# Expert stage pipelined by one tile, with the relu rows turned through DRAM and VectorE instead of on TensorE

## What is computed

```python
kv = einsum('bhsd,bhse->bhde', k, v);  out = einsum('bhsd,bhde->bhse', q, kv)     # 8 batches, 8 heads, 576 x 64
x = out / sqrt(mean(out * out) + 1e-6) * g_norm                                  # -> 4608 tokens x 512
x = square(maximum(x @ w_in, 0)) @ w_out                                         # 512 -> 2048 -> 512
logits = x @ w_gate + modality_bias[modality_id];  e_idx = argmax(logits)        # 8 experts
for e in range(8):                                                               # top-1 routing
    mask = e_idx == e
    out[mask] = gate_w[mask, None] * (maximum(x[mask] @ w1[e], 0) @ w2[e])       # 512 -> 1024 -> 512
```

## Time and profile before

| | |
|---|---|
| runs | 1524.31, 1524.43, 1529.36 us; median 1524.43 |
| profiled execution | span 1524.2 us, 24645 instructions; it has no time of its own beside the span |
| TensorE busy | 97% of the span |
| VectorE, ScalarE, GpSimd busy | 41%, 33%, 24% |
| DMA | 236.42 MB, mean 155 GB/s |
| expert stage | from 1011.6 us to the end |

### The profile page before, as it was taken

The page is one execution under the profiler, slowest core; times in us unless marked ns, Lnnn a source line. Parts: engine busy times, 40 slices in busy tenths (PEclk is TensorE's granted clock), DMA queues, the critical chain, the costliest instruction groups (busy, mean ns, idle before and its releaser), DMA issues.

```text
span 1524.2 us, 24645 instructions
## 1 busy us (share of the span) xinstructions
PE 1478.5 (97%) x7915; PEld 1301.5 (85%) x7916; DVE 619.1 (41%) x1538; ACT 498.7 (33%) x927; POOL 365.0 (24%) x377
## 2 busy tenths in 40 slices
PE   6899999999999999999999999988999999999998
PEld 5788998988999998999898999876888888888886
DVE  3363635445554535453636464422222222222222
ACT  2343433433433333433333433321222222222222
POOL 2452312121312122222222131202222222222221
PEclk8999999999999999999999999999999999999999
DMA  6633655563656463464655354754875112751170
GB/s 155 162 101 118 171 173 162 154 183 92 201 123 209 106 194 123 153 170 156 162 171 160 111 180 151 217 199 156 319 284 182 41 41 78 268 213 41 47 255 21
DMA packets 192772, 236.42 MB, mean 155 GB/s; under 512 B 92287, under 2 KB 107039, under 8 KB 192674
## 3 DMA queue, kind: packets, MB, share of 16 engines
q1 hardware_dynamic: 185122, 215.18, 46.1%
q0 software_dynamic: 7552, 20.03, 3.9%
HBM read 148.14 MB, written 88.07 MB: 155 GB/s over the span
## 4 chain that ended last, share of the span: by engine, by line
PE 85%; DMA 6%; DVE 3%; issue 3%; POOL 2%; ACT 1%; SPq 1%; DVEq 0%; POOLq 0%; ACTq 0%
PE ps_y L810 15%; PE ps_h L810 14%; PE ps_h L632 7%; PE ps_y L632 7%; PE ps_h L634 7%; PE ps_h L633 7%; PE ps_y L634 7%; PE ps_y L633 7%; PE ps_a L668 2%; PE ps_b L695 2%; PE ps_b L717 2%; DMA stage<-in_moe_w_in 2%; DMA w_lo<-stage 1%; PE ps_c L755 1%; PE ps_y L823 1%
## 5 line engine op out<-in xcount | busy, mean ns | idle before, releaser
L543 POOL TENSOR_TENSOR stage<-stage,stage_hi 128x512 f32<-128x512 f32 x128 | 167.6, 1309 | 652.9 <-ACT stage_hi L922 575.0
L1203 DVE TENSOR_TENSOR g_sb<-relu_sb 128x384 f32<-128x384 f32 x192 | 131.5, 685 | 400.1 <-ACT relu_sb L979 395.5
L632 PE MATMUL ps_h<-xT_hi,weights 128*128 128x384 f32 x768 | 268.6, 350 | 5.8 <-POOL weights L535 3.2
L634 PE MATMUL ps_h<-xT_hi,weights 128*128 128x384 f32 x768 | 260.3, 339 | 0.0
L633 PE MATMUL ps_h<-xT_lo,weights 128*128 128x384 f32 x768 | 259.9, 338 | 0.0
L632 PE MATMUL ps_y<-weights,g_hi 128*128 128x512 f32 x576 | 233.8, 406 | 0.3 <-DVE g_lo L1208 0.3
L634 PE MATMUL ps_y<-weights,g_lo 128*128 128x512 f32 x576 | 227.2, 394 | 0.0
L633 PE MATMUL ps_y<-weights,g_hi 128*128 128x512 f32 x576 | 226.0, 392 | 0.0
L979 ACT ACTIVATE relu_sb<-ps_h 128x384 f32<-128x384 f32 x192 | 93.8, 488 | 317.3 <-PE ps_h L634 304.9
L810 PE MATMUL ps_y<-weights,xT_hi 128*128 128x512 f32 x640 | 183.7, 399 | 0.0
L810 PE MATMUL ps_h<-weights,xT_hi 128*128 128x512 f32 x640 | 172.2, 391 | 1.4 <-DVE xT_lo L1106 1.4
(11 more groups left out here) (169 smaller groups left out, 1735.8 us busy)
## 6 DMA issues: line engine op xcount, KB each, us to landing
stage<-in_moe_w SPq DMA_DIRECT2D x128, 256.0 KB, 2.9
w_hi<-stage_hi SPq DMA_DIRECT2D x128, 256.0 KB, 2.8
w_lo<-stage SPq DMA_DIRECT2D x128, 256.0 KB, 3.2
weights<-w_hi SPq DMA_DIRECT2D x32, 1024.0 KB, 6.5
weights<-w_lo SPq DMA_DIRECT2D x32, 1024.0 KB, 6.6
rows<-y_sb SPq DMA_DIRECT2D x13, 774.0 KB, 4.9
k_sb<-in_k SPq DMA_DIRECT2D x60, 144.0 KB, 3.2
v_sb<-in_v SPq DMA_DIRECT2D x30, 288.0 KB, 4.0
```

The lines of the kernel that those rows point to most:

```text
L543: pool.tensor_tensor(stage[n % 2][:, :], stage[n % 2][:, :], stage_hi[n % 2][:, :].bitcast(F32), ALU.subtract).then_inc(piece_lo, 1)
L632: pe.matmul(out_ap, lhs[0], rhs[0], start=start, stop=False)
L634: return pe.matmul(out_ap, lhs[1], rhs[0], start=False, stop=stop)
L1203: dve.tensor_tensor(g_sb[:, :], relu_sb[:, :], relu_sb[:, :], ALU.mult).then_inc(g_done, 1)
```

## The change

What it does, part by part:

1. **Turning h.** `transpose_h` and its four-by-two transposes a tile are gone from TensorE. ScalarE's relu now writes its 512 columns in another order, and ScalarE issues a store of that half to a DRAM buffer `h_dram[half]` (256 KB, runs of 512 bytes) and then a load back (256 KB, 2 KB a partition), which together exchange blocks of rows and columns. VectorE then transposes the 32 x 32 blocks of the 128 x 512 half in one instruction (`turn_h`), and `h_hi` and `h_lo` read that from SBUF instead of PSUM, through a permuted view.
2. **Pipelining.** TensorE's order is hidden(T + 1), output(T) where it was hidden(T), output(T). There is one buffer for the turned h, so `h_hi(T)` waits for output(T - 1). `transpose_rows(T + 1)` now stands in hidden(T), six matmuls before its end. On VectorE `x_lo(T + 1)` stands behind the turn of the first half of tile T, and `scale(T - 1)` behind the turn of the second half. The metadata pass through one more buffer (`meta_mid`).
3. **GpSimd** scatters tile T - 3 where it scattered T - 2, ahead of passing the rows of tile T.
4. **Early tiles and the least number.** `EARLY` goes from 2 to 3, and each expert has at least `LEAST` = 2 tiles. For these inputs: 3 + (2, 2, 3, 13, 3, 10, 2, 3) = 41 tiles, since expert 0 keeps 430 - 384 = 46 tokens for its own tiles and gets 2.
5. **Unrolling.** The loop over pairs of experts becomes eight copies of the code. The waits for weights are one expert's w1 ahead of its first hidden and its w2 behind the first output of that round; expert 1's w2 is loaded without a wait once the lists are in.

The core of the diff (the names and counts of semaphores that follow from it are left out):

```diff
-EARLY = 2
+EARLY = 3
+LEAST = 2
...
+            for e in range(E):
+                n_tiles, previous = tiles_of(eng, e), tile_before(eng, e)
+                at_tile(previous, e, 0)
+                with eng.Fori(1, n_tiles) as t:
+                    at_tile(previous + t, e, t)
...
+            def load_w1(e):
+                if e > 1:
+                    sp.wait_ge(h_ps, tile_before(sp, e - 1) * 2 + (GROUPS * CH + 2))
...
+            def load_w2(e):
+                if e > 1:
+                    sp.wait_ge(y_ps, tile_before(sp, e - 1) + (GROUPS + 1))
...
-            def transpose_h(T, half):
-                pe.wait_ge(relu_done, T * 2 + half + 1)
-                for k_ in range(4):
-                    last = pe.transpose(chunks(ps_hT[half][:, :])[:, k_, :],
-                                        relu_B[half][:, k_ * P:(k_ + 1) * P], ident[:, :])
-                last.then_inc(hT_ps, 1)
...
+            def hidden_of(T, n, at=lambda place: None, rows=True):
                 pe.wait_ge(x_lo_done, T + (ROWS + 1))
                 hidden(n, 0, 0, 6)
                 hidden(n, 0, 6, 3 * KC)
+                hidden(n, 1, 0, 6)
+                if rows:
+                    transpose_rows(T + 1)
+                hidden(n, 1, 6, 3 * KC)
+            def output_of(T, n, at=lambda place: None):
                 pe.wait_ge(y_by_dve, T + GROUPS)
                 pe.wait_ge(hT_lo_done, T * 2 + 1)
+                output(n, 0, 12)
                 pe.wait_ge(hT_lo_done, T * 2 + 2)
+                output(n, 12, 3 * FC)
...
+            hidden_of(0, 0, first_places)
+            hidden_of(1, 0, second_places)
+            output_of(0, 0, second_places)
+            hidden_of(2, 0, third_places, rows=False)
+            output_of(1, 0)
+            transpose_rows(3)
...
+                with pe.Fori(1, n_tiles) as t:
+                    hidden_of(previous + t + 1, e % 2)
+                    output_of(previous + t, e % 2)
+            output_of(last_tile(pe), (E - 1) % 2)
...
+            def store_h(T, half):
+                act.wait_ge(relu_done, T * 2 + half + 1)
...
+                act.dma_start(h_dram[half].rearrange("a p r -> p a r"),
+                              relu_B[half].rearrange("p (a r) -> p a r", a=4)).then_inc(h_out[half], 16)
+            def load_h(previous, half):
+                act.wait_ge(h_out[half], previous * 16 + 32 if previous is not None else 16)
...
+                act.dma_start(h_swapped[half], h_dram[half].rearrange("a (t b) r -> (a t) (b r)", b=4)).then_inc(h_in[half], 16)
...
+                dve.transpose(h_turned[half], h_swapped[half]).then_inc(hT_done, 1)
...
-                act.wait_ge(hT_ps, T * 2 + (half + 1))
+                act.wait_ge(hT_done, T * 2 + (half + 1))
+                act.wait_ge(y_ps, T + GROUPS)
+                act.activation(h_chunks(0, half), turned_chunks(half), ACT.Copy).then_inc(hT_hi_done, 1)
```

More of the change, by code:

```diff
@@ L99, in routed_mlp_program @@
     rows_dram = nc.dram_tensor("rows", [N + 1, ROW], F32, kind="Internal").ap()
+    h_dram = [nc.dram_tensor(f"h_rows{half}", [4, P, P], F32, kind="Internal").ap() for half in range(2)]
     lists_dram = nc.dram_tensor("lists", [EARLY * P + E * LIST, 1], F32, kind="Internal").ap()
@@ L180, in routed_mlp_program @@
         relu_B = [kv_sb[n][:, :, :].rearrange("p a b -> p (a b)") for n in range(2)]
+        h_swapped = [stage_hi[half][:, :].bitcast(F32) for half in range(2)]
+        h_turned = [xn[:, :], tile_T[:, :, :].rearrange("p k t -> p (k t)")]
         W = KC * F
@@ L1001, in relu @@
                 act.wait_ge(h_ps, T * 2 + (GROUPS * CH + half + 1))
-                act.activation(relu_B[half], ps_h[half][:, :], ACT.Relu).then_inc(relu_done, 1)
-            def h_hi(T, half):
-                act.wait_ge(hT_ps, T * 2 + (half + 1))
-                act.activation(h_B[0][:, 4 * half:4 * half + 4, :], chunks(ps_hT[half][:, :]),
-                               ACT.Copy).then_inc(hT_hi_done, 1)
-            def tile(T, e2, n, t):
-                for half in range(2):
-                    relu(T, half)
-                    h_hi(T, half)
-                x_hi(T + 1)
+                if not isinstance(T, int) or T:
+                    act.wait_ge(h_out[half], T * 16)
@@ L1016, in _, with tile @@
+            def tile(previous, e, t, rows=True):
+                T = previous + 1
+                relu(T, 0)
+                store_h(T, 0)
+                relu(T, 1)
+                store_h(T, 1)
+                load_h(previous, 0)
+                if rows:
+                    x_hi(T + 1)
+                load_h(previous, 1)
+                h_hi(T, 0)
+                h_hi(T, 1)
             last_group = Group(0, GROUPS - 1)
             other("yT", 0, None, last_group, True)
+            other("yT", 1, None, last_group, True)
@@ L1018, in _ @@
             relu(0, 0)
-            other("yT", 1, None, last_group, True)
-            h_hi(0, 0)
+            store_h(0, 0)
             other("yT", 2, None, last_group, True)
             relu(0, 1)
+            store_h(0, 1)
+            x_hi(1)
+            load_h(None, 0)
+            load_h(None, 1)
+            other("argmax", 0, None, last_group, True)
+            h_hi(0, 0)
             h_hi(0, 1)
-            other("argmax", 0, None, last_group, True)
-            x_hi(1)
-            for T in range(1, EARLY):
-                tile(T, None, None, None)
+            tile(0, None, None)
@@ L1028, in _ @@
+            tile(1, None, None, rows=False)
+            x_hi(3)
             act.wait_ge(tiles_done, 1)
-            all_experts(act, None, tile)
+            all_experts(act, tile)
         @block.vector
```

274 lines of the change are left out of this document (131 added, 143 removed).

## The result

The changed kernel takes **1685.43 us** (median of 4 runs, 1677.77 to 1695.34), the kernel before beside it 1525.0 us (4 runs): a ratio of **1.105**, 95% interval 1.1004 to 1.1088. The forecast was 1598 us, with a range of 1535 to 1650: slower, as said, but by 160 us and not by 74. The profiled execution took 1677.77 us, its span is 1676.0.

The account below looks back on a forecast made before the run. TensorE's instructions set the pace before; with the change, loops through DRAM would. 1060 to hidden(3) + 190 (11.7 tiles beside weights) + 25.3 x 12.33 = 312 + 10 (clock) + 26 (end) = 1598 us, range 1535 to 1650.

Parts of the forecast that it names:

- 11.36 us of TensorE work: Expert stage: TensorE's own work a tile falls from 12.31 us to 11.36 once two of three transpose groups go.
- Period without weights, 12.33: Loop tiles without weight traffic: 12.33 us each, bounds 11.7 to 13.2, so these tiles gain nothing.
- loop A: Path over x_lo: hidden, relu, half 0's store and load, turn, x_lo, next hidden; 9.42 us plus the load's time.
- loop B: Path over the rows: half 1's store, load, turn, scale, scatter, row copy, row transposes; 6.93 us plus store and load.
- Trips beside weights, +2.0 each: Stores and loads of h while weights stream: 2.0 us longer each, bounds 0 and 3.6, making a tile 16.3 us.
- the 11.7 tiles: Loop tiles run while weights load: 190 us in all at 16.3 us a tile.
- rival 3: Deeper stalls: trips beside weights as slow as the pieces, 19.9 us a tile, 10.8 tiles, 1659 us in all; chance 0.16.
- Clock, 10 us: TensorE's clock halves behind long waits beside weights, adding at most 1.8 us a tile; half taken, 10 us in all.
- Early tiles, h(3) at 1060: Before the loop: hidden(3), whose start is h(3), begins at 1060, losing about 4 us.
- The end, 26.3: From the start of hidden(40), h(40), to the end: 26.3 us, as the last output waits for its own round trip.
- Rival 1: ScalarE's trips aren't slowed by the weights: all 37 periods at 12.33 us, 1540 us in all; chance 0.20.
- Rival 2: Round trip hidden, TensorE's 11.36 us the period: 1502 us; needs store plus load (S + L) at most 4.43; chance 0.07.

Follow-up runs that it names:

- e1: The changed kernel with expert 2 to 7's weight pieces cut from 1 MB to 64 KB, so nearly no weight traffic: 1605.81 us.
- e5: The changed kernel with x_hi ahead of the loads on ScalarE, and x_lo, the metas and scale ahead of both turns on VectorE: 1610.3 us.
- e6: e5 with the weight pieces of experts 2 to 7 cut to 64 KB: 1524.2 us.
- e12: e5 with the edits of e7 and e8, and the weight pieces of experts 2 to 7 cut to 64 KB: 1516.42 us.
- e2: The changed kernel with x_hi ahead of the loads on ScalarE, and x_lo and the metas ahead of the turns on VectorE: 1673.43 us.
- after: The changed kernel itself, without further edits: 1685.43 us, 1.105 times the kernel before.
- e13: e5 with each 1 MB weight piece of experts 2 to 7 as two DMAs of 512 KB, still two in flight: 1588.94 us.
- e8: e5 with expert 1's w2 fetched ahead of the token lists and tile 3's x_hi and x_lo ahead of tile 2's h: 1605.9 us.
- e7: e5 with VectorE's turned halves written to two free PSUM banks instead of SBUF: 1596.1 us.

## Why the prediction was right in direction and wrong in size

The miss is 1676.0 - 1598 = 78 us of span: 4.9 ahead of h(3), 69.7 in the 37 periods (581.7 against 190 + 312 + 10), 3.2 behind h(40). The 69.7 can be split in two ways. By e1, 50 are in the loop without weights and 20 in what the weights add. By kind, TensorE's waits are 115.8 us where the forecast's terms leave 82 (512 - 420.3 - 10), and its work is 45.5 us slower where 10 were set down: 34 and 35.5. So the loops were too short in the sum, and the clock term was too small; each is half of the miss.

- **What bounds the kernel; 11.36 us of TensorE work.** Right: 11.4 in e5, e6 and e12.
- **The chain is the question, not the sum of work.** Right. VectorE is at 42%; its 0.71 us turn was taken as 0.69.
- **Period without weights, 12.33.** This step failed first, and is the larger part. The structure was right (A and B, of nearly equal length; e2), but the sum let B, 12.33, be the longer, and A is what TensorE waits for. In the tile shown loop A takes 12.99 us where the sum gave 9.42 + 2.6 = 12.02: +7.78 to the load's issue for 7.25 (TensorE's hidden takes 6.24 behind a wait, not 5.92; the steps in the queue are longer than 0.08), 2.98 from the load's issue to VectorE's release for 2.6 (half 1's loads alone do land after 2.6; half 0's goes out 0.7 us behind half 1's store), and 0.1 until VectorE starts. Then the mean: in e1, without weight traffic, it is 13.7: half 0's load takes 3.3 us to its turn in the median and up to 5.7, as trips also meet GpSimd's row transfers and each other, and two loops without slack let each such delay through. What delays a single trip is read from the order of transfers, not isolated by a run; e6 shows that with slack nearly none of it reaches TensorE (0.3 us of waits in its 37 periods). 37 x (13.67 - 12.33) = **50 us**, of which 30 are waits and 20 slower work of TensorE. The bound of 13.2 was there, and was still too low for a mean.
- **Trips beside weights, +2.0 each.** Failed: the stores behind a group of pieces take 5.1 to 7.9 us in after's chain, and half 0's loads up to 9.2 (8.74 and 7.20 in e5's), up to 5 or 6 more than in quiet. The bound "as slow as a piece, 6.5" was exceeded. That a trip waits for the pieces ahead of it and then makes its own fits the tile shown and e13, but no run shows it alone. With it the 11.7 tiles failed: 19 periods are long, 17 with pieces in flight, since each expert comes as two groups of pieces, and a group touches more than one tile. But the long tile itself, 17.9 us with its slower work, is between the forecast's 16.3 (without it) and rival 3's 19.9. In all the weights cost 76 us (after less e1) where 190 + 10 - 11.7 x 12.33 = 56 were forecast: **20 us**. Of these 20, 16 are slower work and only 4 are waits (50 against 46): the longer trips don't add up so far, since their waits fall on one tile and spare the next (6.2, 3.4, 9.0 and 1.6 us in the four from h(4) on), and the mean wait of a long tile is 4.7 us where 16.3 - 11.36 = 4.9 were forecast. That this comes out so near is luck.
- **Clock, 10 us.** Right in kind: 0.50 behind a long wait. Failed in size: it costs 35 us in the 37 periods. The step that failed is "In loop B only 1.83 us of TensorE's work lies on the path, so a halved clock adds at most 1.8 us a tile". That holds for loop B; in loop A, which TensorE waits for, the whole of hidden is on the path, and hidden(5) takes 9.12 us of work for 6.06, 3.1 more. And it comes in 15 stretches, where 11.7 tiles were reckoned. Some 10 us more of slower work stand at full clock, about 0.3 behind each wait; nothing here says why.
- **Early tiles, h(3) at 1060.** 1064.9, and near by luck: the last logits, from which the forecast counts, come 8.5 us earlier in this run than before (1012.13 for 1020.65), in code that the change doesn't touch. From there to h(3) are 52.7 us and not 39.4: 31.7 for 28.2 to the turned ids, 21.0 for 11.2 behind them. Named there: the row transposes, the round trip, the ids. Not named: ScalarE's loads for tile 2 stand ahead of tile 3's `x_hi`, and half 1's load is issued only when its store has landed beside expert 1's w2. e8, which sets both right, takes 12.5 us behind the ids, but its ids come later by nearly as much.

```profile
1012.13 0.96 PE L717 MATMUL ps_b<-wg_sb,tile_T 128*128 128x8 f32 x8
...
1043.81 0.74 PE L875 MATMUL ps_b<-ident,stage 96*128 96x96 f32 x3 [5.56 <-DMA stage<-lists]
...
1050.81 6.51 ACTq L1018 DMA_DIRECT2D stage_hi<-h_rows  x2
...
1064.86 1.65 PE L810 MATMUL ps_h<-weights,xT_hi 128*128 128x512 f32 x3 [9.29 <-DVE xT_lo L1134]
```

- **The end, 26.3.** 29.5. The last output waits 3.1 us and runs its first matmuls at half clock:

```profile
1661.30 2.08 PE L810 MATMUL ps_y<-weights,xT_hi 128*128 128x512 f32 x4 [3.13 <-DVE xT_lo L1255]
```

- **The rivals.** Rival 1 (weights don't slow ScalarE's trips) is excluded by e1. Rival 2 (hidden) needed S + L under 4.43 and falls; but e6 and e12 show that the same trips are hidden by another order. Rival 3 (deeper stalls, 1659) was the nearest, and still 17 us short: its 10.8 loaded tiles were too few, and its 19 us for the clock too.
- **Order of causes**, by what undoing one gives: VectorE's and ScalarE's order 70 (after to e5; 54 in waits, 16 in slower work), or 83 without weights (e1 to e6); the weights 76 with the change's order (e1), 89 with e5's (e6); they don't add, because the order's slack takes up part of a trip and the weights take it away again.

## What to carry to other kernels

Before a transfer is put into a loop, ask what stands behind its wait on each in-order engine: here `x_lo` and `scale` cost more by standing behind the returning h than the transposes saved. Price a round trip through DRAM by its length beside the largest transfers that the same event releases, twice, and set it against the time the consumer really leaves; pipelining by one tile gave 10.6 us, enough for 6 and not for 16. And where TensorE waits on a loop, count the matmuls on the path behind the wait at the lower clock: that was 35 us here, as much as the transposes saved. And where the whole gain is 35 us of 1524, count the fill and the drain of the deeper pipeline first.

## What the runs showed of the hardware

- ScalarE's 256 KB loads land after 2.6 us in quiet (the eight of half 1 between 1240 and 1350 us: 2.6 at least and at most; half 0's have no landing time in the trace). A store issued 0.7 us behind 2 MB of pieces of another engine takes 7.6 us in the tile shown and the load behind it 6.2; in e5's chain they take 8.7 and 7.2. By the Trainium skill's "DMA: Bandwidth & Descriptors", section "Issuing engines are not separate DMA queues", the queues share the same 16 DMA engines; the trace agrees, with these numbers.
- A tile of 128 x 512 f32 read in the turned order costs 1.1 us from SBUF (after) and 0.60 (ScalarE) or 0.69 (VectorE) from PSUM (e7).
- TensorE's granted clock fell to 0.50 in 15 stretches of the 37 periods of after, each behind a wait of 2.1 us or more, and in none in the kernel before, which never waits there. Hidden then takes up to 9.12 us of work instead of 6.06.
- Where `h_lo` reads two operands in SBUF, GpSimd's scatter beside it sometimes takes twice as long: 37 scatters of e1, minimum, median and maximum ns, then all 41 of e7, which has one operand in PSUM:

```profile
L593 POOL DMA_INDIRECT out<-q_sb,meta_i x37: 1004/1004/2042, 1068.2 to 1565.4; - x37
...
L593 POOL DMA_INDIRECT out<-q_sb,meta_i x41: 967/1001/1017, 1054.0 to 1589.7; - x41
```

  In e5's order it is mostly `h_lo` that is held up: half 0's starts beside GpSimd's copy of the rows and takes 1.50 us in the median, and 0.69 in e7, where the same order reads PSUM. One of them in e5:

```profile
1274.48 0.67 POOL L584 COPY k_sb<-k_sb 128x516 f32<-128x516 f32 x1
1274.54 1.50 DVE L1255 TENSOR_TENSOR xT_lo<-xn,xT_hi 128x512 fp32r<-128x512 f32 x1 [0.71 <-ACT xT_hi L1023]
```

  By the Trainium skill's "SBUF — State Buffer", section "SBUF: two separate sides", a VectorE operation with two SBUF inputs and a GpSimd one that reads SBUF lock each other out for a whole instruction. The rows agree with it, and e7, whose expectation set out to test it, takes both away.
- VectorE's 32 x 32 block transpose of 128 x 512 f32 takes 0.70 to 0.71 us into SBUF (after) and 0.68 to 0.73 into PSUM (e7).
